# Gather and scatter that read the index table in place, and the second expert's weights asked for at once

## The reference, cut to what matters

```
attn = attention(q, k, v, tau)                 # 4 x 8 heads, 576 x 64 each
x = attn as 2304 tokens x 512
x = relu(x @ w_in)**2 @ w_out                  # one MLP of 2048 for all tokens
logits = x @ w_gate;  e_idx = argmax(logits)   # one of 8 experts for each token
gate_w = softmax(logits)[e_idx];  eom = sigmoid(x @ w_output_gate)
for e in range(8):
    mask = e_idx == e
    out[mask] = gate_w * eom[mask, e] * (relu(x[mask] @ w1[e]) @ w2[e])
```

## Time and profile before

| | |
|---|---|
| median of three runs | 1134.29 us |
| the profiled execution | 1132.23 us |
| its span, first to last instruction | 1130.5 us |
| the expert stage in it | from 786 us to the end |
| PE (TensorE matmul) busy | 1046.8 us, 93% |
| DVE (VectorE) busy | 678.1 us, 60% |
| ACT (ScalarE) busy | 556.1 us, 49% |
| POOL (GpSimd) busy | 495.1 us, 44% |
| mean granted TensorE clock | 0.977 of full speed |

### The profile page before, as it was taken

The page is one execution under the profiler, slowest core; times in us unless marked ns, Lnnn a source line. Parts: engine busy times, 40 slices in busy tenths (PEclk is TensorE's granted clock), DMA queues, the critical chain, the costliest instruction groups (busy, mean ns, idle before and its releaser), DMA issues. The chain is left out here.

```text
span 1130.5 us, 22630 instructions
## 1 busy us (share of the span) xinstructions
PE 1046.8 (93%) x8153; PEld 925.7 (82%) x8153; DVE 678.1 (60%) x1336; ACT 556.1 (49%) x854; POOL 495.1 (44%) x734
## 2 busy tenths in 40 slices
PE   7999999999989999999899999997489999999995
PEld 5778787877769999999899989996377777777774
DVE  5887887878756534334334433433667777777773
ACT  4777777778753211211121112111367777777773
POOL 4777777777740000000000000000548888888973
PEclk9999999999999999999999999998599999999999
DMA  4323232232112100000000000002492573411100
GB/s 105 79 63 80 50 86 55 67 76 64 37 49 76 29 20 1 25 1 19 2 24 1 19 2 24 1 19 71 151 394 94 179 254 106 178 39 37 38 27 22
DMA packets 76314, 75.40 MB, mean 67 GB/s; under 512 B 48815, under 2 KB 54959, under 8 KB 76210
## 3 DMA queue, kind: packets, MB, share of 16 engines
q1 hardware_dynamic: 72690, 63.49, 18.4%
q0 software_dynamic: 3520, 10.49, 2.7%
HBM read 64.52 MB, written 10.49 MB: 66 GB/s over the span
## 5 line engine op out<-in xcount | busy, mean ns | idle before, releaser
L820 ACT ACTIVATE r_buf<-h_ps 128x288 f32<-128x288 f32 x128 | 52.6, 411 | 347.3 <-PE h_ps L777 347.3
L884 DVE TENSOR_TENSOR r_buf<-r_buf 128x288 f32<-128x288 f32 x128 | 58.7, 458 | 243.5 <-ACT r_buf L820 243.5
L1169 POOL MEMSET ones<- 128x128 bf16 x1 | 0.2, 209 | 453.0 <-POOLq L637 453.0
L1097 DVE TENSOR_TENSOR w_lo<-w_experts,w_hi 128x2048 fp32r<-128x2048 f32 x66 | 163.4, 2501 | 32.1 <-ACT w_hi L1336 32.1
L1336 ACT ACTIVATE w_hi<-w_experts 128x2048 fp32r x88 | 163.4, 1909 | 32.1 <-issue 14.0
L777 PE MATMUL h_ps<-x_hi,w_in_hi 128*128 128x288 f32 x512 | 154.4, 302 | 6.1 <-DVE x_lo L878 3.5
L777 PE MATMUL h_ps<-x_hi,w_in_lo 128*128 128x288 f32 x512 | 151.9, 297 | 3.1 <-issue 3.1
L777 PE MATMUL h_ps<-x_lo,w_in_hi 128*128 128x288 f32 x512 | 152.4, 298 | 0.0
L796 PE MATMUL y_ps<-g_hi,w_out_hi 128*128 128x288 f32 x512 | 151.4, 296 | 0.3 <-DVE g_lo L890 0.3
L796 PE MATMUL y_ps<-g_hi,w_out_lo 128*128 128x288 f32 x512 | 151.1, 295 | 0.0
L796 PE MATMUL y_ps<-g_lo,w_out_hi 128*128 128x288 f32 x512 | 151.0, 295 | 0.0
(11 more groups left out here) (196 smaller groups left out, 2407.0 us busy)
## 6 DMA issues: line engine op xcount, KB each, us to landing
w_experts<-in_moe_w_dram SPq DMA_DIRECT2D x16, 2048.0 KB, 13.9
k_raw<-in_k_dram SPq DMA_DIRECT2D x32, 128.0 KB, 3.1
q_raw<-in_q_dram SPq DMA_DIRECT2D x32, 128.0 KB, 3.0
w_raw<-in_moe_w_in_dram SPq DMA_DIRECT2D x16, 256.0 KB, 3.2
v_nat<-in_v_dram SPq DMA_DIRECT2D x16, 256.0 KB, 2.6
y_T<-in_moe_w_out_dram SPq DMA_DIRECT2D x16, 256.0 KB, 2.7
y_rows<-y_row SPq DMA_DIRECT2D x16, 256.0 KB, 2.2
v_odd<-in_v_dram SPq DMA_DIRECT2D x16, 64.0 KB, 2.3
```

What stands on the lines that cost most here:

```text
L820: nc.scalar.activation(r_buf[f % 2][:], h_ps[f % 2][:, 0:HALF], ACT.Relu).then_inc(relu_done, 1)
L884: nc.vector.tensor_tensor(r[:], r[:], r[:], ALU.mult).then_inc(g_ops, 1)
L1097: alu.tensor_tensor(group_of(w_lo, g), raw_group(buf, g), group_of(w_hi, g).bitcast(F32), ALU.subtract).then_inc(done, 1)
L1169: nc.gpsimd.memset(ones[:], 1.0).then_inc(pool_set, 1)
```

## The change

Four things are edited, all in `experts`.

1. `read_token`, `write_token`, `name_tokens` and their semaphores are gone. Both indirect DMAs take their index straight from the column of `place_token`.
2. GpSimd's loop over slots is written out, since the column is named when the program is built. With it go the counting of passed waits (`pool_on`) and the loop's register arithmetic.
3. GpSimd's second wait for `hi_done` in `split` is gone; `split_lo` waits for the same value.
4. SyncE asks for expert 1's weights right after expert 0's, ahead of the first announcement and ahead of the wait for the gathers. Expert 2's stay behind that wait.

```diff
+            for e in range(BUFS - 1):
+                load(e)
             announce(0)
             for p in range(RING):
                 sp.wait_ge(gathered[p], 16)
-            for e in range(1, BUFS):
-                load(e)
+            load(BUFS - 1)
...
-            def name_tokens(column, t, named):
-                nc.gpsimd.tensor_copy(column[:], place_token[:, ds(t, 1)]).then_inc(named, 1)
-                wait_first(pool, named, t + 1, pool_on)
...
+            def gather(t):
+                if t >= RING:
+                    pool.wait_ge(xt_set, t + 1 - RING)
+                nc.gpsimd.indirect_dma_start(x_g[t % RING][:], None, y_rows[:, :],
+                                             bass.IndirectOffsetOnAxis(ap=place_token[:, t:t + 1], axis=0)
+                                             ).then_inc(gathered[t % RING], 16)
+            def store(t):
+                pool.wait_ge(scaled, t + 1 + RING)
+                nc.gpsimd.indirect_dma_start(out[:, :], bass.IndirectOffsetOnAxis(ap=place_token[:, t:t + 1], axis=0),
+                                             o_sb[t % RING][:], None, bounds_check=TOK - 1, oob_is_err=False
+                                             ).then_inc(stored[t % RING], 16)
             def split(t):
                 buf = weight_buffer(pool, t)
-                wait_first(pool, hi_done, 4 * t + 4, pool_on)
                 split_lo(pool, nc.gpsimd, t, 3, buf, lo_pool)
...
-            with pool.Fori(0, FULL // RING - 1) as i:
-                for p in range(RING):
-                    gather(RING * i + p + RING, p)
-                    store(RING * i + p, p)
-                    split(RING * i + p + 1)
+            for t in range(FULL - RING):
+                gather(t + RING)
+                store(t)
+                split(t + 1)
```

More of the change, by code:

```diff
@@ L987, in experts @@
         place_factor = sb("place_factor", [P, SLOTS])
-        read_token = [sb(f"read_token{p}", [P, 1], I32) for p in range(RING)]
-        write_token = [sb(f"write_token{p}", [P, 1], I32) for p in range(RING)]
         w_raw = sb("w_experts", [P, BUFS * WE])
@@ L1053, in experts @@
         stored = [sem(f"stored{p}") for p in range(RING)]
-        pool_on = sem("experts_pool_passed")
         sp_on = sem("experts_sp_passed")
         act_on = sem("experts_act_passed")
-        read_named, write_named = sem("read_named"), sem("write_named")
         block = ctx.enter_context(nc.Block())
@@ L1122, in announce @@
                 sp.sem_inc(w2_ready, 1)
-            load(0)
+            for e in range(BUFS - 1):
+                load(e)
             announce(0)
@@ L1189, in _ @@
             for t in range(RING):
-                gather(t, t)
+                gather(t)
             pool.wait_ge(control_done, 1)
             split(0)
-            with pool.Fori(0, FULL // RING - 1) as i:
-                for p in range(RING):
-                    gather(RING * i + p + RING, p)
-                    store(RING * i + p, p)
-                    split(RING * i + p + 1)
+            for t in range(FULL - RING):
+                gather(t + RING)
+                store(t)
+                split(t + 1)
             used = slots_used(pool)
@@ L1205, in if_used @@
                         work(t)
-            for t in range(RING * (FULL // RING - 1), SLOTS):
-                if_used(t + RING, lambda t: gather(t, t % RING))
-                if_used(t, lambda t: store(t, t % RING))
+            for t in range(FULL - RING, SLOTS):
+                if_used(t + RING, gather)
+                if_used(t, store)
                 if_used(t + 1, split)
```

## The result

The changed kernel takes 1114.88 us, the median of four runs from 1111.03 to 1117.24, beside 1134.15 us for the kernel before: a ratio of 0.983 with a 95% interval from 0.980 to 0.986. That is 19.3 us faster, where 22.3 were forecast; the interval reaches from 16 to 23 us. The profiled execution, of 1115.11 us, spans 1113.4 us against 1130.5, 17.1 us less.

What follows compares the result with a forecast made beforehand. The prediction took turns between GpSimd and VectorE's two-input splits as the bound, 13.82 us a slot, with TensorE next at 12.74. Gains of 3.98 + 1.66 + 16.9 + 0.2 - 0.4 = 22.3 us gave 1112.0 us, range 1107.5 to 1119.

Steps and rivals of the forecast that it cites:

- the price of the copies: Expert slots 2 to 20: removing both copies takes a slot from 13.82 to 12.88 us, 16.9 us in all.
- The loop written out: GpSimd's slot loop: its register work lies beside running splits, so 0 us, bounds 0 and +1.
- The early weights: Expert 1's load: gains 3.98 us at slot 1 and 1.66 at the next turn, costs 0.4 at the first gather.
- part 1: Expert stage: the copies for gather and scatter go; slots 2 to 20 gain 16.9 us.
- the meeting: First gather's last 3.5 us lie beside the early load's tail, ending by 809.3; cost 0 to 0.9 us, taken as 0.4.
- the reading by which the gather gets its share at once: First gather: DMA engines serve queues in turn, packet by packet, so the early load's cost is nearer 0.
- R1: Rival, start: first gather stays in the load's crowd for 8.9 us, slot 0 is 4.3 later, 1116 us; chance 0.12.
- R2: Rival, scatter: register work runs after VectorE's split, turns stay within 0.1 of 13.8 us, gain 4.4, 1130; chance 0.07.
- R3: Rival, gather: it holds VectorE's first split up by 0.85 us, turns of 13.7, gain 6, 1128; chance 0.07.
- R4: Rival, scatter: index read in place lengthens each scatter's 0.90 us; at three times that, 1148 us; chance 0.06.
- The end: Last scatter: only its copy goes, gaining 0.2 us; the last slot is TensorE's and unchanged.
- The sum: Whole kernel: 3.98 + 1.66 + 16.9 + 0.2 - 0.4 = 22.3 us gained, median 1112.0 us.

Runs made afterwards that it cites:

- e8: The changed kernel with GpSimd leaving out two of its group's four rows from slot 1 on, no usable kernel: 1110.07 us, 12.72 us a slot.
- e4: The changed kernel with both index copies and the waits for them back, loop still written out and weights early: 1131.06 us, ratio 0.998.
- e11: The changed kernel with only the scatter's copy and its wait back, behind the wait for the scale: 1129.12 us, 13.75 us a slot.
- e2: The kernel before with only SyncE's edit, expert 1's weights asked for right after expert 0's: 1131.57 us, ratio 0.9985.
- e3: The changed kernel with SyncE's early weights undone, so only copies gone and slots written out: 1116.81 us, ratio 0.986.
- e1: The changed kernel run once more without any edit: 1116.76 us, ratio 0.986.
- e5: The changed kernel with only w1 of expert 1 asked for early, w2 after the first gather has landed: 1113.65 us, ratio 0.981.
- e6: The changed kernel with GpSimd's split of the next slot put ahead of the scatter's store: 1107.58 us, ratio 0.978.
- e12: The changed kernel with only the scatter's copy and its wait back, ahead of the wait for the scale, a buffer per slot: 1115.16 us.

## Why the prediction was right, and where it was off

**What bounds the kernel, and the price of the copies: right.** Not 4.29 us a slot but 0.9. GpSimd's splits from slot 2 to slot 20 were forecast 12.88 apart and came 12.93 apart: 16.0 us gained of 16.9. The working held in its parts: scatter 0.89 after VectorE's third split (0.90 forecast), the beat of two slots 25.83 us (25.75). How a beat divides was off: 12.76 and 13.07, where I had 12.84 and 12.9. VectorE's pair starts 0.18 before GpSimd's split ends in the one (865.36 against 865.54) and 0.16 after it in the other (852.60 against 852.44), so the longer turn is longer by 0.33, where I had allowed 0.15 beyond 12.75. The bound was TensorE against GpSimd in a tie, as e8 shows from the one side (12.72 without GpSimd) and e4 from the other (13.76 with the copies).

**The loop written out: put at nothing, and it was not quite nothing.** e4 gives 0.06 us a slot, about 1 us over the slots 2 to 20. Of the 0.9 us a slot the scatter's copy is 0.82 (e11) and the loop the rest.

**The early weights: the term was mis-sized.** I gave them 3.98 us in slot 1 and 1.66 in slot 2 and took 0.4 off. Alone they gained 0.9 (e2), on top of the other part 0.1 to 1.2 (e3 against the changed kernel and e1). The sum for the start came nearer than its terms: from `place_token` to the end of GpSimd's split of slot 2 the changed kernel takes 4.4 us less, and I had 5.2. Two errors. First, the working of slot 1 used the scatter without its copy, so most of what I wrote down for the weights belonged to part 1: alone, that part gained 3.3 us by slot 3. Second, the price was too low: the first hidden layer came 1.1 to 1.3 us later, not 0.4, and 1.0 to 2.3 later over all ten kernels of the table that ask for both of expert 1's weights at once. Why it differs so much among them no run shows. Windows of the changed kernel:

```profile
808.00:810.00 2.00, 0.00 (x0) 0.00 (x0) 1.57 (x1) 1.61 (x1) 1.70 (x2) 0.50 1.05 410
810.00:812.00 2.00, 0.00 (x0) 0.00 (x0) 2.00 (x2) 0.00 (x0) 1.70 (x2) 0.50 0.58 231
```

The load runs at its full rate (410 GB/s in the first window) past the gather's issue at 807.36 and ends at about 811.1, 4.3 after `place_token`, where I had 4.0. TensorE took up the gathered rows at 812.59, 5.23 after the issue; before the change that was 3.68 (806.09 to 809.77). So the meeting was right and its end nearly, but TensorE took up the rows 1.4 after the load's end, and the gather was issued 0.25 earlier than before, not 0.5. VectorE's pair, which I had as cover, ended at 812.93, and the low part of the transposed rows behind it had to wait until 814.37. e5 confirms the cause: with the load's second half out of the way the rows are used 3.72 after the issue and the first hidden layer comes at 6.74 again. So the reading by which the gather gets its share at once and costs nearly nothing did not come true. This is R1 in part, a quarter to a half of its price of 4.3. Its sign, `hidden` of slot 0 later than 813.5, did appear: 815.12, and 813.6 without the 1.5 that came ahead of the stage. `hidden` of slot 1, forecast for 826.7, began at 829.53: 1.5 from ahead of the stage, 0.9 from this price beyond the 0.4, and 0.4 in slot 0.

**The rivals.** R2 (the wait only moves): false, the scatter starts 0.9 into VectorE's third split. R3 (the gather goes first): false; gather and pair both start at 852.60 and neither stands. The Trainium skill (SBUF — State Buffer, Who interferes with whom) says that whichever starts first holds the SBUF ports that both share for the whole instruction. The trace agrees for a split against a split (6.37 us instead of 4.6 for GpSimd's in e6) and for a DMA caught by a split, but here an indirect DMA and a two-input split started together and both ran at their own length, and in e6 the scatter starts some 0.73 us ahead of VectorE's pair (940.07 and 940.80), which still takes 4.49 to 4.50. R4 (reading in place is dear): false; the scatter ends 0.89 after the split whether it reads in place (changed kernel) or from its own tile (0.90).

**The end.** 0.25 us gained for 0.2 forecast. What followed the last scatter took 1.76 longer. The changed kernel's scatter left stragglers, here from 1106.5 to 1108.5 us, where its other packets had ended by 1106.5:

```profile
DMA packets 5, 0.02 MB, mean 8 GB/s; under 512 B 1, under 2 KB 1, under 8 KB 5
```

The end comes in two kinds across the table, 7.2 to 7.9 and 9.0 to 9.3 us, and the same kernel shows both (e1 has 7.46, the changed kernel 9.27). So it is not the change, but it hit this profile. What holds the stragglers up is open.

**The sum.** Forecast by slot 20's split were 22.5 less 0.4, 22.1 us; measured were 20.2, from `place_token` to the hidden layer of slot 21. Of the 5.2 us between the forecast 22.3 and the profile's 17.1, 2.0 are this shortfall and 3.3 are the 1.5 ahead of the stage and the 1.8 after it, neither of which is the change. The medians hold such chance too: 19.3 us here, 16.7 in e1.

## What to carry to other kernels

Read a busy GpSimd beside VectorE's timeline before pricing its instructions: a 2 us copy of 128 elements was 0.18 us of work and a place in a queue. What such an instruction costs is decided by which instruction of the other engine it meets and by what waits behind it, so moving it (e12) or moving its neighbour (e6) can be worth as much as deleting it. When a bound is taken away, work out the next one to the same precision: here it stood 1.1 us behind, so taking out 4.3 us of copies could bring no more than that.

## What the runs showed of the hardware that I had not expected

- The prediction had one row for an indirect DMA caught by VectorE's two-input split. Every slot of the changed kernel shows it now: the scatter ends 0.87 to 0.90 us after the split. The other way round no profile here shows a split held up: beside a gather that ran at the same time the pair took 4.49 to 4.54 us, and 4.49 or 4.50 alone.
- TensorE's clock comes back at different points after slot 0 has begun. Windows of the changed kernel, whose hidden layer began at 815.12:

```profile
816.00:818.00 2.00, 2.00 (x6) 1.52 (x6) 1.72 (x1) 1.94 (x2) 0.00 (x0) 0.50 0.29 35
818.00:820.00 2.00, 2.00 (x10) 1.61 (x9) 0.57 (x1) 0.28 (x1) 1.86 (x1) 0.89 0.94 350
```

and of e1, where it began at 816.07:

```profile
818.00:820.00 2.00, 2.00 (x6) 1.59 (x5) 1.52 (x1) 0.89 (x1) 0.91 (x1) 0.50 0.71 145
820.00:822.00 2.00, 2.00 (x6) 1.54 (x5) 0.00 (x0) 0.41 (x1) 2.00 (x1) 0.50 1.01 408
822.00:824.00 2.00, 2.00 (x12) 1.64 (x12) 0.00 (x0) 0.49 (x2) 1.94 (x1) 1.00 1.02 420
```

  It was at its lower level for 3.3 us of work in the one (0.89 in the window from 818 puts the rise at 818.4) and 5.9 in the other, and slot 0 took 14.41 and 15.63 us. In the kernel before it fell again around the gap of 2.2 us ahead of slot 1 (0.50 in the window from 830 to 832); where that gap is gone, so is the fall.
- Kernels that are the same up to the expert stage differ by 5.5 us there (803.5 to 809.0). That, and the two kinds of end, are why medians 2 us apart say little here and the stretches of the table say more.
